# Top-32 attention: scores formed twice, once with keys on partitions and masked there by TensorE in PSUM

## The reference

```python
batch, n_heads, seq, head_dim = (4, 8, 576, 64)
...
scores = scale * np.matmul(q, k.transpose(0, 1, 3, 2))
kth = np.partition(scores, -top_k, axis=-1)[..., -top_k:-top_k + 1]
mask = scores >= kth
scores = np.where(mask, scores, -1000000000.0)
scores = scores - np.max(scores, axis=-1, keepdims=True)
attn = np.exp(scores)
attn = attn / (np.sum(attn, axis=-1, keepdims=True) + 1e-09)
return np.matmul(attn, v).astype(np.float32)
```

## Time and profile before

| | |
|---|---|
| three runs | 1195.18, 1195.63, 1196.86 us (median 1195.63) |
| the profiled execution | 1195.35 us, span 1193.4 us |
| TensorE, busy in the span | 1008.1 us (84%) |
| VectorE | 820.3 us (69%) |
| GpSimd | 601.6 us (50%) |
| ScalarE | 580.5 us (49%) |
| mean granted clock of TensorE | 0.948 |

### The profile page before, as it was taken

How to read it: one execution, slowest core, us unless ns; L and a number is a source line. 1 busy time by engine, 2 the same in 40 slices (tenths; PEclk the granted TensorE clock), 3 DMA queues, 4 the chain that set the end, 5 groups by cost and what they waited for, 6 DMA issues and landing times. The chain is left out here.

```text
span 1193.4 us, 25656 instructions
## 1 busy us (share of the span) xinstructions
PE 1008.1 (84%) x6763; PEld 890.6 (75%) x6763; DVE 820.3 (69%) x3417; ACT 580.5 (49%) x1474; POOL 601.6 (50%) x571
## 2 busy tenths in 40 slices
PE   6877877787787888888584689999999999999995
PEld 5766766676776777777453688988989889898874
DVE  6999999999999999999598334335244352443523
ACT  5877877787776777777431222222122121331211
POOL 5888888888888888888453201111111111441101
PEclk9999999999998998999887689999999999999997
DMA  3011110011110011100081300000100002120000
GB/s 85 2 32 33 32 32 22 11 32 31 32 31 11 21 32 31 31 11 1 3 301 71 106 19 9 28 18 18 35 15 20 18 18 105 29 76 10 18 19 7
DMA packets 38189, 43.47 MB, mean 36 GB/s; under 512 B 24785, under 2 KB 24785, under 8 KB 38098
## 3 DMA queue, kind: packets, MB, share of 16 engines
q1 hardware_dynamic: 34738, 32.06, 8.8%
q0 software_dynamic: 3360, 10.49, 2.6%
HBM read 70.84 MB, written 9.96 MB: 68 GB/s over the span
## 5 line engine op out<-in xcount | busy, mean ns | idle before, releaser
L284 POOL TENSOR_TENSOR rests<-score,work 128x576 f32<-128x576 f32 x144 | 233.3, 1620 | 86.3 <-DVE work L537 86.3
L603 PE MATMUL bank<-v_sb,prob_t 128*128 128x129 f32 (+1 forms) x1440 | 229.3, 300 | 0.0
L481 DVE MAX8 cand<-score 128x8 f32<-128x72 f32 x1152 | 214.6, 216 | 5.9 <-ACT score L353 5.7
L603 PEld LDWEIGHTS bank<-v_sb,prob_t 128*128 128x128 f32 (+1 forms) x1440 | 197.6, 204 | 19.8 <-issue 3.6
L297 POOL TENSOR_TENSOR prob<-prob,rests 128x576 f32<-128x576 f32 x144 | 203.6, 1414 | 0.7 <-DVE rests L541 0.7
L593 PE MATMUL bank<-ident,prob 128*128 128x128 f32 x576 | 99.8, 298 | 110.5 <-POOL prob L297 110.2
L593 PEld LDWEIGHTS bank<-ident,prob 128*128 128x128 f32 x576 | 63.8, 146 | 142.7 <-POOL prob L297 139.9
L381 ACT ACTIVATE prob_t<-bank 128x512 f32<-128x512 f32 x144 | 86.1, 598 | 103.0 <-PE bank L594 102.5
L1139 POOL TENSOR_SCALAR stat<-stat 128x1 f32<-128x1 f32 x20 | 4.5, 227 | 212.6 <-DVE stat L1294 212.6
L367 ACT ACTIVATE prob<-score,neg_max 128x576 f32<-128x576 f32 x144 | 110.5, 767 | 0.1
L523 DVE MAX8 top<-rests 128x8 f32<-128x576 f32 x144 | 109.0, 757 | 1.9 <-POOL rests L284 1.4
(11 more groups left out here) (189 smaller groups left out, 2650.3 us busy)
## 6 DMA issues: line engine op xcount, KB each, us to landing
raw<-w SPq DMA_DIRECT2D x22, 2048.0 KB
q_raw<-q_t SPq DMA_DIRECT2D x16, 320.0 KB, 2.9
k_raw<-k_t SPq DMA_DIRECT2D x16, 288.0 KB, 2.7
v_sb<-v SPq DMA_DIRECT2D x32, 128.0 KB, 2.3
x_rows<-x_n SPq DMA_DIRECT2D x16, 256.0 KB
win_sb<-w_in SPq DMA_DIRECT2D x1, 2048.0 KB, 7.9
wout_sb<-w_out SPq DMA_DIRECT2D x1, 2048.0 KB, 13.7
v_sb<-v SPq DMA_DIRECT2D x32, 16.0 KB, 2.2
```

Source lines behind the costliest of these rows:

```text
L284: pool.tensor_tensor(rests[:, s % 2, :], score[:, s % SB, :], work[:, b, :], ALU.mult).then_inc(rested, 1)
L481: ins = dve.max(cand[:, s % 2, 8 * c:8 * c + 8], score[:, s % SB, c * CW:(c + 1) * CW])
L603: last = pe.matmul(out_ps[s % 2], prob_t[0:k, s % 2, c, :], v_sb[par][0:k, c, :], start=(c == 0), stop=(c == KC - 1))
```

## The change

`stage_a` is parted in two. `attend_again`, the slow pass, is what the second call was. `attend_quick` is new:

- q and k are used as f32, without splitting. Scores are formed for a *unit* of two tiles: the same query chunk of both heads, (0, 1), (2, 3), (4, 5), (6, 7), and the shared tile 8 alone. Products for the two heads alternate, on rows 0 to 63 and 64 to 127.
- VectorE's last operation writes `drop` in bf16: 1 for a score that falls away, 0 for a kept one, plus `shift`, the row's maximum over 2048.
- TensorE forms the scores again with keys on partitions (`turned_scores`, 64 rows) and adds to them, in the same place in PSUM, the product of `drop` and -2048 times the identity (`drop_unkept`, bf16, 128 rows). The result is the score less the maximum, and 2048 less where it is dropped.
- ScalarE takes one exponential of 128 x 640 out of PSUM, which gives the turned probabilities. The exponential from SBUF, both copies after the transposes, the transposes and GpSimd's product by the mask are gone. GpSimd keeps only `rests`.
- VectorE's chain runs two tiles ahead, its candidates three, where before it was one and two.
- The check also asks that no shift is above 1. Loads of a pair's q, k and v wait for the values of the pair two before.

```diff
+UNITS = [(2 * c, 2 * c + 1) for c in range(FULL)] + [(2 * FULL,)]
+UNITS_AHEAD = 3
+DROPS = 6
+OUT_OF_REACH = 2048.0
...
+            attend_quick(nc, q_t, k_t, v, psum, ident, x_all, locals())
+            check_quick(nc, bank, ident, low, high, again)
+            attend_again(nc, q_t, k_t, v, bank, ident, x_all, locals())
...
+def attend_quick(nc, q_t, k_t, v, psum, ident, x_all, g):
+    score_ps = [psum[:, 2 * i:2 * i + 2, 0:HALF] for i in range(2)]
+    turned_ps = psum[:, 4:7, :].rearrange("p b f -> p (b f)")
+    out_ps = [psum[:, 7, i * OW:i * OW + VW] for i in range(2)]
+    turned_at = (0, 2 * BANK - P)
+    place = ([0, 1, 2, 3, 4], [1, 2, 3, 4, 0])
...
+            load_qk(0, 0)
+            load_v(0, 0)
+            sp.wait_ge(qk_loaded, 32)
+            load_qk(1, 1)
+            sp.wait_ge(v_loaded, 64)
+            load_v(1, 1)
+            for_later()
+            with sp.Fori(1, PAIRS // 2) as m:
+                for par in range(2):
+                    i = m * 2 + par
+                    hold(sp, (summed, (m * 2 + (par - 1)) * NT), (qk_loaded, i * 32), (v_loaded, i * 64))
+                    load_qk(i, par)
+                    load_v(i, par)
...
+            def rest(t, s):
+
+                hold(pool, (below_ready, t + 1), (rest_found, t - 1))
+                pool.tensor_tensor(rests[:, s % 2, :], score[:, s % SB, :], work[:, s % 2, :], ALU.mult).then_inc(rested, 1)
...
+            def scale_max(t, s):
+
+                act.wait_ge(max_found, t + 1)
+                at_least(act, kept, t - WRAP + 1)
+                act.activation(shift[:, s:s + 1], top[:, s % SB, 0:1], ACT.Copy, scale=1.0 / OUT_OF_REACH).then_inc(shift_ready, 1)
...
+            def exp(t, s):
+                act.wait_ge(masked, t + 1)
+                at_least(act, summed, t - 1)
+                at = turned_at[s % 2]
+                act.activation(prob_t[:, s % 2, :, :].rearrange("p c q -> p (c q)"), turned_ps[:, at:at + QW], ACT.Exp,
+                               scale=SCALE).then_inc(exped, 1)
...
+            def pair(i, par, more):
+                left = WRAP if more else WRAP - par * NT
+                for n, unit in enumerate(UNITS):
+                    for j in unit:
+                        t, s = i * NT + j, par * NT + j
+                        if j == unit[-1]:
+                            if left - unit[0] > UNITS_AHEAD * 2 - 1:
+                                ahead = n + UNITS_AHEAD
+                                base = ahead // len(UNITS) * NT
+                                for k in UNITS[ahead % len(UNITS)]:
+                                    save_scores(i * NT + base + k, (par * NT + base + k) % WRAP)
+                            for k in unit:
+                                exp(i * NT + k, par * NT + k)
+                        if left - j > 3:
+                            count(t + 3, (s + 3) % WRAP)
+                        if left - j > 4:
...
+                    hold(dve, (sure_found, c + 1), (rested, c - 1), (counted, c - 1))
+                    dve.tensor_scalar(work[:, sc % 2, :], score[:, jc, :], top[:, jc, SURE - 1:SURE], None,
+                                      ALU.is_lt).then_inc(below_ready, 1)
+                if rest:
+                    hold(dve, (picked, t + 1), (shift_ready, t + 1), (exped, t - DROPS + 1))
+                    dve.tensor_scalar(drop[:, s % DROPS, 0:S], score[:, s % SB, :], thr[:, s:s + 1], shift[:, s:s + 1],
+                                      ALU.is_lt, ALU.add).then_inc(kept, 1)
...
+            def scores(i, par, unit):
+                last = i * NT + unit[-1]
+                pe.wait_ge(qk_loaded, (i + 1) * 32)
+                at_least(pe, saved, last - 1)
+                for half in range(2):
+                    for j in unit:
+                        s, c = par * NT + j, j // 2
+                        ins = pe.matmul(score_ps[s % 2][:, half, :], q_sb[par][rows_of(j), c * P:(c + 1) * P],
+                                        k_sb[par][rows_of(j), half * HALF:(half + 1) * HALF], start=True, stop=True)
+                        if half == 1:
+                            ins.then_inc(scored, 1)
+
+            def turned_chunk(s, c):
+                at = turned_at[s % 2] + place[s % 2][c] * P
+                return turned_ps[:, at:at + P]
+
+            def turned_scores(par, s, j, c):
+                return pe.matmul(turned_chunk(s, c), k_sb[par][rows_of(j), c * P:(c + 1) * P],
+                                 q_sb[par][rows_of(j), j // 2 * P:(j // 2 + 1) * P], start=True, stop=False)
+
+            def drop_unkept(s, c):
+                return pe.matmul(turned_chunk(s, c), drop[:, s % DROPS, c * P:(c + 1) * P], minus_far[:, :], start=False, stop=True)
+
+            def masked_scores(i, par, unit):
+
+                t, s, last = i * NT + unit[0], par * NT + unit[0], len(unit) - 1
+                at_least(pe, exped, t)
+                pe.wait_ge(kept, t + last + 1)
+                turned_scores(par, s, unit[0], FULL)
+                drop_unkept(s, FULL).then_inc(tail_masked, 1)
+                for c in range(FULL):
+                    if last and c == FULL - 1:
+                        pe.wait_ge(tail_masked, i * len(UNITS) + unit[0] // 2 + 1)
+                        turned_scores(par, s + 1, unit[1], FULL)
+                        drop_unkept(s + 1, FULL)
+                    for n, j in enumerate(unit):
+                        turned_scores(par, s + n, j, c)
+                    for n, j in enumerate(unit):
+                        ins = drop_unkept(s + n, c)
+                ins.then_inc(masked, len(unit))
+
+            def values(i, t, par, s):
+                pe.wait_ge(exped, t + 1)
+                pe.wait_ge(v_loaded, (i + 1) * 64)
+                at_least(pe, out_saved, t)
+                for c in range(KC):
+                    k = P if c < FULL else TAIL
+                    ins = pe.matmul(out_ps[s % 2], prob_t[0:k, s % 2, place[s % 2][c], :], v_sb[par][0:k, c, :],
+                                    start=(c == 0), stop=(c == KC - 1))
+                ins.then_inc(summed, 1)
+
+            def pair(i, par, more):
+                last = par == 1 and not more
+                for n, unit in enumerate(UNITS):
+                    ahead = n + UNITS_AHEAD
+                    if ahead < len(UNITS):
+                        scores(i, par, UNITS[ahead])
+                    elif not last:
+                        scores(i + 1, 1 - par, UNITS[ahead - len(UNITS)])
+                    masked_scores(i, par, unit)
+                    for j in unit:
+                        values(i, i * NT + j, par, par * NT + j)
+
+            pe.wait_ge(pads_set, 5)
+            pe.wait_ge(far_set, 1)
+            for n in range(UNITS_AHEAD):
+                scores(0, 0, UNITS[n])
+            all_pairs(pe, pair)
```

More of the change, by code:

```diff
@@ L87, in build_program @@
         x_rows = nc.dram_tensor("x_rows", (N + 1, D), F32).ap()
-        bank = [ctx.enter_context(nc.psum_tensor(f"bank{i}", [P, 2, BANK], F32)) for i in range(4)]
+        psum = ctx.enter_context(nc.psum_tensor("psum", [P, 8, BANK], F32))
+        bank = [psum[:, 2 * i:2 * i + 2, :] for i in range(4)]
         ident = sb(ctx, "ident", [P, P])
@@ L182, in stage_a @@
         prob = sb("prob", [P, PB, S])
-        rests = sb("rests", [P, 2, S])
-        unread = sb("unread", [P, S], mybir.dt.bfloat16)
-        cand = sb("cand", [P, 2, CAND])
-        below = sb("below", [P, PB])
-        pick = sb("pick", [P, TOPK - SURE + 1])
-        thr = sb("thr", [P, 2 * NT])
         prob_t = sb("prob_t", [P, 2, KC, P])
@@ L277, in low_k @@
                                    ALU.subtract).then_inc(k_split, 1)
-            def rest(t, s):
-                b = s % PB
-                pool.wait_ge(below_ready, t + 1)
-                at_least(pool, masked, t - 1)
-                pool.tensor_tensor(rests[:, s % 2, :], score[:, s % SB, :], work[:, b, :], ALU.mult).then_inc(rested, 1)
             def mask(t, s):
                 b = s % PB
-                if quick:
-                    keeps = rests[:, s % 2, :]
-                else:
-                    keeps = score[:, s % SB, :]
-                    hold(pool, (ranked, t + 1), (exped, t + 1))
-                    pool.tensor_scalar(keeps, score[:, s % SB, :], top[:, s % SB, TOPK - 1:TOPK], None,
-                                       ALU.is_ge).then_inc(kept, 1)
+                keeps = score[:, s % SB, :]
+                hold(pool, (ranked, t + 1), (exped, t + 1))
+                pool.tensor_scalar(keeps, score[:, s % SB, :], top[:, s % SB, TOPK - 1:TOPK], None,
+                                   ALU.is_ge).then_inc(kept, 1)
                 pool.wait_ge(kept, t + 1)
@@ L301, in pair @@
                     t, s = i * NT + j, par * NT + j
-                    if quick and (more or s < 2 * NT - 1):
-                        rest(t + 1, (s + 1) % (2 * NT))
                     mask(t, s)
@@ L368, in exp @@
```

(11 more changed lines are left out.)

325 lines of the change are left out of this document (205 added, 120 removed).

## The result

| | |
|---|---|
| four runs of the changed kernel | 1383.8, 1385.09, 1400.55, 1411.67 us (median 1392.82; of the first three 1385.09) |
| kernel before, same session | 1195.41 us (median of 4) |
| ratio | 1.163, 95% interval 1.153 to 1.174 |
| forecast | 1291 us, range 1195 to 1370 |

The change makes the kernel slower, as forecast, but by 190 to 197 us in place of 96, beyond the upper end of the range.

The account below looks back on a forecast made before the run. The prediction took VectorE to bound the kernel at 3.86 us a tile, and TensorE after the change. TensorE's later end (+90 us), loop stalls (6) and check (1), taken as 96 on 1195.35, gave 1291 us, range 1195 to 1370.

Parts of the forecast that it names:

- TensorE becomes the bound: Attention: TensorE needs 9.09 us a unit against 2 x 3.60 for VectorE, so TensorE sets the pace; +90 us.
- The sum for a unit: TensorE's work and waits for a full unit of two tiles in attention: 9.09 us.
- the three terms: Masked scores of a unit on TensorE: products on turned operands 1.76, drops 0.6, turns inside 1.84 us.
- the turn: TensorE switching between 128 and 64 array rows: 0.14 us one way, 0.2 the other, 14 in two tiles.
- The exponential wait: TensorE waits before a unit's values for the exponential it just fed: 0.77 plus 0.13 for hand-overs, 0.9 us.
- The single tile: TensorE's work on the shared tile that stands alone at a pair's end, exponential included: 5.0 us.
- The terms behind the sum: Added to the whole kernel: TensorE's later end 90 us, stalls between loop pairs 6, check operations 1; summed as 96.
- All from rows at the full granted clock: TensorE slot prices in attention, read at full clock: f32 record of 129 columns 0.11 us, fp32r of 288 0.13.
- a rival, at 0.91 and 45 us: TensorE's granted clock in attention falls to 0.91: +45 us, total 1336; chance 0.10.
- The halves overlap fully: Products on different array halves run wholly side by side: 0.69 us less a unit, total 1247; chance 0.15.
- No overlap: f32 products on different array halves never run at once: 1.19 us more a unit, total 1367; chance 0.12.
- VectorE stays the bound: Attention: turns under 0.07 us leave VectorE setting the pace, 37 us won, total 1158; chance 0.17.

Follow-up runs that it names:

- experiment 11: Experiment 5 with ScalarE copying new scores right behind the unit's exponentials and saved output, a unit further ahead, nine score buffers for six: 1170.02 us, ratio 0.981.
- experiment 3: The changed kernel plus 12 unread bf16 products behind each unit's masked scores, where TensorE waited for the exponential: 1302.21 us, ratio 1.091.
- experiment 6: Experiment 2 with all products of one head in front of those of the other: 1274.68 us, ratio 1.066.
- experiment 2: The changed kernel with each unit's ten turned products first, then its ten drops, 2 turns in place of 11: 1235.82 us, ratio 1.035.
- experiment 1: The changed kernel with values one unit late, behind the next unit's masked scores, and scores ahead between the two tiles: 1264.23 us, ratio 1.061.
- 4: The changed kernel with the scores ahead placed between the values of the unit's two tiles, exponential wait kept: 1326.24 us, ratio 1.111.
- experiment 5: The changed kernel with drops grouped and values one unit late, scores ahead between the values: 1208.16 us, ratio 1.011.
- experiment 9: Experiment 5 plus 16 unread bf16 products behind each unit's values: 1200.44 us, ratio 1.006.

## Why the direction was right and the size wrong

**TensorE becomes the bound: right.** The profile after shows VectorE in 59 waits on saved scores, 234.9 us in all, and GpSimd's product by the mask is gone. VectorE alone would have been quicker: `pick` 0.215 us (forecast 0.21), `work` 0.504 (0.50). Its drop took 0.576 us as a median where I kept 0.51; that lies within the bounds. A step without a wait is 3.57 us (drops at 306.47, 310.04, 313.61), against 3.60; where VectorE really was the bound (experiment 11) the mean step was 3.65.

```profile
306.47 0.58 DVE L410 TENSOR_SCALAR drop<-score,thr,shift 128x576 bf16<-128x576 f32 x1
...
310.04 0.57 DVE L410 TENSOR_SCALAR drop<-score,thr,shift 128x576 bf16<-128x576 f32 x1
```

**The sum for a unit: right, by errors that cancel.** 8.90 against 9.09 us. That they are so near is luck: a wait that was left out (0.50) stands against turns priced too high. From 343.22 to 344.51 the scores take 1.3 us (forecast 5 slots, 1.25). The masked scores with their turns take about 3.7 (344.51 to 348.2) where the three terms made 1.76 + 0.6 + 1.84 = 4.2. The term that was too high is the turn: a single tail, two slots of 0.11 and a turn to 128 rows, takes 0.31 (344.51 to 344.82), so the turn is 0.09; two drops and a turn back take 0.21 (345.41 to 345.62), 0.09 again, where I had 0.14 and 0.2. A chunk pair without its turn is 0.43 - 0.09 = 0.34 (344.98 to 345.41): three slots, as forecast. The exponential wait is 0.79 (0.9), the values without their wait 2.64 (340.08 to 343.22, less 0.50; forecast 2.74). The 0.50 us for the saved output was not foreseen: the values ask for the output of the tile just before (`out_saved` at t), where those of the kernel before ask for the one before that (t - 1). ScalarE stands idle for the first tile's values, copies them, and only then can TensorE go on at 342.15:

```profile
341.78 0.23 ACT L319 ACTIVATE x_all<-psum 128x65 f32 x1 [0.41 <-PE psum L483]
```

The order rows showed the wait on `out_saved`, but I took it as already met. Nor was the wait for `v_sb` foreseen, 8.5 us in all. The single tile came out at 5.05 us (5.0). The terms behind the sum, 90 + 6 + 1, make 97 and not 96, which changes nothing.

**"All from rows at the full granted clock": this is the step that failed.** The slot prices were those of the upper level, and the sum used them for all of attention. The loss to the clock stood at nothing in the sum and had only a rival, at 0.91 and 45 us, with a chance of 0.10 (I took the level of the earlier trace rows over, as if it belonged to the chip and not to the order of work). Measured: 0.82 over 20 to 820 us, and 83 us by the medians of experiment 3 (102.6 by its profile), about twice what the rival said. Experiment 3 shows it, since a unit at the upper level is 8.90 us in both kernels. With the clock nearly full the change takes 1302 us, 11 over the forecast. By the profile of experiment 3 the first unit ran at the lower level (its turned products at 21.50, the next unit's at 36.87: 15.4 us), and a pair without a stretch at the lower level took 40.8 to 42.6 us (41.5).

The Trainium skill (TensorE: Matmul & The Clock Gate, "A second HAM failure mode: psum-queue depth-cycling") tells of a kernel whose short idle times between groups of products make the clock swing between its levels. This trace agrees: the clock swings between 1.00 and 0.50 with regular waits of 0.79 and 0.50 us. I had not weighed that rule.

**The rivals.** "The halves overlap fully" would have made a chunk pair two slots, and it has three. "No overlap" would have made it four, and experiment 6, with the heads apart, is slower than experiment 2. "VectorE stays the bound" needed turns under 0.07 us; they are 0.09, close, but the 0.50 us wait and the clock would have spoiled it too.

**What the change could have given.** Its idea on VectorE was priced at 37 us, and experiment 11 gets 23 by the medians (25 by the ends of attention, 565.3 against 590.2): TensorE's work has to be ordered in few turns (experiment 2), its waits on ScalarE have to lie beside work (1, 4), and the scores have to reach VectorE (11). The forecast saw the turns and the exponential; it said that nothing could be put in the gap "since the scores ahead were issued in front of it", which is true of this order and false of the design.

## What to carry to other kernels

When an engine becomes the bound, look for the prices of its instructions at both levels of its clock and ask what the new order does to the level; here 1.3 us of waits in a unit of 9 came with a mean of 0.84, and the clock cost as much again as the waits themselves (83 us, and 64 x 1.29 = 83). Group products by the rows of the array that they use, and place behind an instruction whose result another engine must handle the work that doesn't need it. When an engine waits for a copy, look at the queue of the engine that makes it: the scores of experiment 5 were ready and stood behind counts, and that reordering, with the buffers it needs, brought the last 38 us.

## What the runs showed of the hardware

- The clock fell to its lower level with TensorE busy 86% of the time (448 of 520 us) and regular waits of only 0.79 and 0.50 us. Twelve products a unit that nobody reads brought it back to 0.98 and made the kernel 83 us shorter.
- No single count orders the runs. Experiment 3 keeps the eleven turns and the 64-row products and has 0.98; experiment 9 keeps waits for drops (52.6 us in 51 pieces) and has 0.99, with two turns and 16 unread products a unit; experiment 2 keeps both regular waits and has 0.94; experiment 1 has all the turns and only 34.5 us of waits for drops, is busy 95%, and has 0.90. So waits matter, and what of the order (the turns, the 64-row products) makes them matter more was not tried apart and stays open.
- f32 products of 64 rows that alternate between the halves of the array follow at 0.059 to 0.064 us a record (experiment 2); grouped by halves, at (2.05 - 0.27) / 19 = 0.094 (experiment 6).
- A turn between 64-row and 128-row products costs 0.09 us in either direction in the trace of the change.
- VectorE's comparison with a second operation and a bf16 output takes 0.576 us where one operation with an f32 output takes 0.504, both over 576 columns: the narrower output made it no faster in sum. The two differences were not tried apart.
